# RWKV attention with two MoE layers on one core: r's odd columns read in place by the first level's matmuls, and the order of VectorE's steps changed

## What is computed

```python
for t in range(S):                       # attention with a decaying state
    cur = einsum('bhd,bhe->bhde', u * k[t], v[t])
    y[t] = einsum('bhd,bhde->bhe', r[t], state + cur)
    state = w[t][..., None] * state + einsum('bhd,bhe->bhde', k[t], v[t])
x = relu(y @ w_in) ** 2 @ w_out          # dense MLP, 384 -> 2048 -> 384
out = gate * (relu(x[e] @ w1[e]) @ w2[e])  # top-1 of 8 experts, 384 -> 1024 -> 384
```

## Time and profile before

| | |
|---|---|
| three runs, us | 453.21, 453.87, 456.42 (median 453.87) |
| the profiled execution, us | 453.21 |
| its span in the profile, us | 451.2 |
| mean granted clock of PE | 0.997 |
| DMA | 63.39 MB, mean 140 GB/s |

### The profile page before, as it was taken

The page is one execution under the profiler, slowest core; times in us unless marked ns, Lnnn a source line. Parts: engine busy times, 40 slices in busy tenths (PEclk is TensorE's granted clock), DMA queues, the critical chain, the costliest instruction groups (busy, mean ns, idle before and its releaser), DMA issues.

```text
span 451.2 us, 14525 instructions
## 1 busy us (share of the span) xinstructions
PE 427.7 (95%) x5882; PEld 405.8 (90%) x5882; DVE 303.3 (67%) x763; ACT 257.5 (57%) x527; POOL 57.1 (13%) x77
## 2 busy tenths in 40 slices
PE   2689999999999999999999999999999899999994
PEld 2578999999999999999999999998997789999994
DVE  4787956667777867786868638658548877677510
ACT  2265866446654665466556565574548876586421
POOL 7400000000000100010001000211030333321201
PEclk9999999999999999999999999999999999999998
DMA  8817795870220123000000085522885998520001
GB/s 275 290 52 257 275 315 204 286 303 4 98 99 3 37 74 124 1 26 15 3 3 20 21 293 199 175 89 67 308 266 156 333 336 277 195 62 2 30 2 44
DMA packets 35643, 63.39 MB, mean 140 GB/s; under 512 B 3981, under 2 KB 21951, under 8 KB 35569
## 3 DMA queue, kind: packets, MB, share of 16 engines
q1 hardware_dynamic: 33264, 57.88, 37.5%
q0 software_dynamic: 2304, 4.47, 2.7%
HBM read 50.77 MB, written 14.19 MB: 144 GB/s over the span
## 4 chain that ended last, share of the span: by engine, by line
PE 87%; issue 3%; DVE 3%; ACT 3%; DMA 3%; SPq 1%; POOLq 0%; DVEq 0%; ACTq 0%
PE bank L719 22%; PE bank L705 22%; PE pair L626 6%; PE bank L932 6%; PE bank L885 5%; PE pair L590 4%; PE pair L885 3%; PE pair L900 3%; PE bank L939 3%; PE bank L900 3%; PE pair L645 2%; PE pair L680 1%; DMA KS<-in_krw 1%; DMA stage<-in_moe_w_in 1%; PE pair L657 1%
## 5 line engine op out<-in xcount | busy, mean ns | idle before, releaser
L705 PE MATMUL bank<-XH,W 128*128 128x256 f32 x576 | 118.7, 284 | 0.1
L719 PE MATMUL bank<-W,GH 128*128 128x384 f32 x372 | 98.3, 345 | 0.0
L705 PEld LDWEIGHTS bank<-XH,W 128*128 128x128 f32 x576 | 94.9, 189 | 1.1 <-issue 0.4
L705 PE MATMUL bank<-XL,W 128*128 128x256 f32 x288 | 80.6, 280 | 0.0
L1277 DVE TENSOR_TENSOR GL<-GG,GH 128x256 fp32r<-128x256 f32 x96 | 40.3, 419 | 34.5 <-ACT GH L971 34.2
L1075 ACT ACTIVATE RB<-bank 128x256 f32<-128x256 f32 x96 | 36.6, 381 | 46.6 <-PE bank L705 46.0
L719 PEld LDWEIGHTS bank<-W,GH 128*128 128x128 f32 x372 | 61.7, 188 | 1.2
L719 PE MATMUL bank<-W,GL 128*128 128x384 f32 x186 | 62.6, 337 | 0.0
L971 ACT ACTIVATE GH<-GG 128x256 fp32r<-128x256 f32 x96 | 40.2, 418 | 34.8 <-PE bank L719 33.0
L1214 DVE TENSOR_TENSOR KS<-KS 128x512 f32<-128x512 f32 x72 | 49.6, 690 | 8.1 <-PE pair L626 8.0
L705 PEld LDWEIGHTS bank<-XL,W 128*128 128x128 f32 x288 | 54.3, 189 | 0.0
(11 more groups left out here) (164 smaller groups left out, 710.2 us busy)
## 6 DMA issues: line engine op xcount, KB each, us to landing
raw<-in_moe_w SPq DMA_DIRECT2D x23, 768.0 KB, 7.4
stage<-in_moe_w SPq DMA_DIRECT2D x9, 768.0 KB, 7.9
KS<-in_krw SPq DMA_DIRECT2D x12, 512.0 KB, 6.1
slots<-X SPq DMA_DIRECT2D x8, 579.0 KB, 6.3
VV<-in_v SPq DMA_DIRECT2D x12, 288.0 KB, 7.0
KS<-in_krw SPq DMA_DIRECT2D x12, 256.0 KB, 6.3
stage<-in_moe_w_in SPq DMA_DIRECT2D x4, 768.0 KB, 7.3
stage<-in_moe_w_out SPq DMA_DIRECT2D x4, 768.0 KB, 6.6
```

The costliest lines, as they stand in the source:

```text
L705: last = nc.tensor.matmul(bank[4 + f % 2][:, 0:2 * P], win[wa][:, c, f * P:(f + 1) * P], xa[:, c, :], start=n == 0, stop=n == 3 * KM - 1)
L719: last = nc.tensor.matmul(bank[6 + m][:, 0:DM], ga[(NF * g + f) % G3][:, cols], wout[wa][:, f, :], start=f == 0 and n == 0, stop=f == NF - ...
```

## The change

- `mixed_copied` copies only k's even columns into `MIX` (256 elements per partition). `first_level` takes as moving operand the 32 even columns of `UT` and then the 32 odd columns of r where they were loaded, so the first level's columns come out evens first, then odds; PE waits for the load as well.
- `first_select` writes `AD` and reads `eye` (now laid out [C / 2, 2]) with a stride of 2, to undo that order. POOL builds `eye` in two instructions.
- `update` of level 0 waits for the first level's matmuls (which still read r), so `first_select` stands ahead of it. `next_totals` goes into `update`, and `upd` is raised by the totals instead of by the update; DVE waits for `tot` only in block 0. The waits for `made` and `cleared` move ahead of the pipeline.
- `level` uses n = 64 stationary columns for levels 1 to 4 (32 for level 5, as before).

```diff
--- before.py
+++ after.py
@@ -115,7 +115,7 @@
         GL = [sb(f"GL{n}", [P, 2 * P], F32R, on=p1) for n in range(G3)]
         mask2 = IN[0][0][:, :, :].rearrange("p h n -> p (h n)")[:, 0:NMASK * C].rearrange("p (l n) -> p l n", l=NMASK)
         mask = sb("mask", [P, NMASK, C // 2], on=p1)
-        eye = sb("eye", [P, C], on=p1)
+        eye = sb("eye", [P, C // 2, 2], on=p1)
         U = sb("U", [P, HP], on=p1)
         empty = X2[:, 0, :]
         X2B = sb("X2B", [P, 2, ROW], on=p1)
@@ -355,10 +355,6 @@
             first = off[l] - off[1]
             return UT[t][i % 2][:, first:first + (XW >> l)] if l else KRW[t][i % 2][:, 2 * XW:3 * XW]
 
-        def every_second(first, apart):
-
-            return bass.AP(first.tensor, first.offset, [first.ap[0], [apart, 2], [2, XW // 2]])
-
         def left_right(x):
             return x.rearrange("p (g two o) -> p two g o", two=2, o=1)
 
@@ -507,11 +503,11 @@
                                                pattern=[[2 * L, C // L], [0, L]], channel_multiplier=-1)
             step(last)
             pool.wait_ge(cst, n_cst[0])
-            step(nc.gpsimd.tensor_tensor(eye[:, :], ident[:, 0:C], ident[:, C:P], ALU.add))
+            step(nc.gpsimd.tensor_tensor(eye[:, :, 0], ident[:, 0:C:2], ident[:, C:P:2], ALU.add))
+            step(nc.gpsimd.tensor_tensor(eye[:, :, 1], ident[:, 1:C:2], ident[:, C + 1:P:2], ALU.add))
             step(nc.gpsimd.tensor_tensor(mask[:, :, :], mask2[:, :, 0:C // 2], mask2[:, :, C // 2:C], ALU.add))
             pool.wait_ge(cst, n_cst[0])
-            odd = right_half(eye[:, :], 0)[:, :, 0]
-            nc.gpsimd.tensor_tensor(odd, odd, mask[:, 0, :], ALU.add).then_inc(made, 1)
+            nc.gpsimd.tensor_tensor(eye[:, :, 1], eye[:, :, 1], mask[:, 0, :], ALU.add).then_inc(made, 1)
 
             def first_totals(t, l):
 
@@ -600,6 +596,7 @@
 
             def first_level(i, t):
 
+                pe.wait_ge(ld_kr[t][i % 2], 16 * (i // 2 + 1))
                 pe.wait_ge(mixed_raw[t], i + 1)
                 pe.wait_ge(mixed_u[t], i + 1)
                 need(pe, xl_ready[t], i)
@@ -607,8 +604,10 @@
                     for h in range(2):
                         for a in range(2):
                             rows, c = slice(DP * a, DP * a + D), q * P + h * C
-                            last = nc.tensor.matmul(pair[t][half(h, a), a, q * P:q * P + C], MIX[t][rows, c:c + C],
-                                                    UT[t][i % 2][rows, c:c + C], start=q == 0, stop=q == HP - 1)
+                            even = UT[t][i % 2][rows, c:c + 1]
+                            reads = bass.AP(even.tensor, even.offset, [even.ap[0], [XW + 1, 2], [2, C // 2]])
+                            last = nc.tensor.matmul(pair[t][half(h, a), a, q * P:q * P + C], MIX[t][rows, c:c + C], reads,
+                                                    start=q == 0, stop=q == HP - 1)
                 last.then_inc(att[t], 1)
 
             def level(i, t, l):
@@ -617,7 +616,7 @@
                 if t == 0 and i >= 3 and l == NL - 1:
                     pe.wait_ge(rank_used, i - 2)
                 x = KRW[t][i % 2]
-                n = C - (1 << l)
+                n = C if l < NMASK else C // 2
                 for q in range(HP):
                     for h in range(2):
                         for a in range(2):
@@ -973,8 +972,7 @@
             def mixed_copied(i, t):
                 act.wait_ge(ld_kr[t][i % 2], 16 * (i // 2 + 1))
                 need(act, inc_done[t], i)
-                copy(every_second(UT[t][i % 2][:, 1:2], (2 - i % 2) * WIDTH - 1),
-                     every_second(KRW[t][i % 2][:, 1:2], XW - 1)).then_inc(mixed_raw[t], 1)
+                copy(MIX[t][:, 0:XW:2], KRW[t][i % 2][:, XW:2 * XW:2]).then_inc(mixed_raw[t], 1)
 
             def level_blocks(i, t):
                 act.wait_ge(att[t], NSTEP * i + NL)
@@ -1193,42 +1191,40 @@
 
                 dve.wait_ge(ld_kr[t][i % 2], 16 * (i // 2 + 1))
                 need(dve, inc_done[t], i)
-                out = every_second(UT[t][i % 2][:, 0:1], (2 - i % 2) * WIDTH + 1)
-                x = every_second(KRW[t][i % 2][:, 0:1], XW + 1)
-                tt(out.rearrange("p r (q n) -> p r q n", q=HP), x.rearrange("p r (q n) -> p r q n", q=HP),
+
+                def both(first, apart):
+                    return bass.AP(first.tensor, first.offset, [first.ap[0], [apart, 2], [P, HP], [2, C]])
+
+                tt(both(UT[t][i % 2][:, 0:1], (2 - i % 2) * WIDTH + 1), both(KRW[t][i % 2][:, 0:1], XW + 1),
                    U[:, :].rearrange("p (r q n) -> p r q n", r=1, n=1).to_broadcast([P, 2, HP, C]),
                    ALU.mult).then_inc(mixed_u[t], 1)
 
             def update(i, t, l):
                 L = 1 << l
+                n = XW // (2 * L)
+                dve.wait_ge(att[t], NSTEP * i + l + 1)
                 if l == 0:
                     dve.wait_ge(ld_wd[t][i % 2], 16 * (i // 2 + 1))
-                    dve.wait_ge(mixed_raw[t], i + 1)
                     dve.wait_ge(mixed_u[t], i + 1)
                 else:
-                    dve.wait_ge(att[t], NSTEP * i + l + 1)
                     dve.wait_ge(upd[t], NL * i + l)
-                    dve.wait_ge(tot[t], NL * i + l)
+                if i == 0:
+                    need(dve, tot[t], l)
+                td = left_right(totals(i, t, l))
                 x = halves(i, t, l)
-                td = left_right(totals(i, t, l))
-                tt(x, x, td.to_broadcast([P, 2, XW // (2 * L), L]), ALU.mult).then_inc(upd[t], 1)
-
-            def next_totals(i, t, l):
-
+                last = tt(x, x, td.to_broadcast([P, 2, n, L]), ALU.mult)
                 if i > 0:
-                    td = left_right(totals(i, t, l))
-                    tt(totals(i, t, l + 1), td[:, 0, :, 0], td[:, 1, :, 0], ALU.mult).then_inc(tot[t], 1)
+                    last = tt(totals(i, t, l + 1), td[:, 0, :, 0], td[:, 1, :, 0], ALU.mult)
+                last.then_inc(upd[t], 1)
 
             def first_select(i, t):
 
                 dve.wait_ge(att[t], NSTEP * i + 1)
-                if i == 0:
-                    dve.wait_ge(made, 2)
-                    dve.wait_ge(cleared, 2)
+                got = pair[t][:, :, :].rearrange("p a (q c) -> p (a q) c", q=HP)[:, :, 0:C]
                 nc.vector.copy_predicated(
-                    AD[t][:, :, :],
-                    eye[:, :].bitcast(U32).rearrange("p (x n) -> p x n", x=1).to_broadcast([P, H, C]),
-                    pair[t][:, :, :].rearrange("p a (q c) -> p (a q) c", q=HP)[:, :, 0:C]).then_inc(sel[t], 1)
+                    AD[t][:, :, :].rearrange("p x (n b) -> p x b n", b=2),
+                    eye[:, :, :].bitcast(U32).rearrange("p (x n) b -> p x b n", x=1).to_broadcast([P, H, 2, C // 2]),
+                    got.rearrange("p x (b n) -> p x b n", b=2)).then_inc(sel[t], 1)
 
             def select(i, t, l):
                 L = 1 << l
@@ -1251,14 +1247,17 @@
             def scale_start(i, t):
 
                 if not opens(i, t):
-                    dve.wait_ge(tot[t], NL * (i + 1))
+                    dve.wait_ge(upd[t], NL * i + NL)
+                    if i == 0:
+                        dve.wait_ge(tot[t], NL)
                     need(dve, end_ready, 2 * i + t)
                     tt(heads(SD[:, :]), heads(start_state(i, t)), decay(i, t, 0), ALU.mult).then_inc(mid_scaled, 1)
 
             def state(i, t):
                 n = 2 * i + t
                 dve.wait_ge(inc_ready[t], i + 1)
-                dve.wait_ge(tot[t], NL * (i + 1))
+                if i == 0:
+                    dve.wait_ge(tot[t], NL)
                 if not opens(i, t):
                     dve.wait_ge(mid_scaled, n + 1 - opened(i, t))
                     tt(states(i, t)[:, 0], SD[:, :], states(i, t)[:, 0], ALU.add).then_inc(mid_ready, 1)
@@ -1402,13 +1401,10 @@
                 if (n, t, k) == (0, 0, 0):
                     mixed_weighted(0, 1)
                 if k == 0:
-                    update(n, t, k)
                     first_select(n, t)
-                else:
-                    if k < NMASK:
-                        select(n, t, k)
-                    update(n, t, k)
-                next_totals(n, t, k)
+                elif k < NMASK:
+                    select(n, t, k)
+                update(n, t, k)
 
             def body(i, attn, mlp, gate):
                 for s in range(NF):
@@ -1463,6 +1459,8 @@
                 nc.vector.memset(AD[t][:, :, :], 0.0).then_inc(cleared, 1)
             dve.wait_ge(ld_u, 16)
             mixed_weighted(0, 0)
+            dve.wait_ge(made, 2)
+            dve.wait_ge(cleared, 2)
             pipeline(dve, body)
 
             def first_rows_low(q):
```

## The result

The changed kernel takes 458.49 us in the median of 14 runs, the kernel before 453.99 beside it: the ratio is 1.0091, with a 95% interval of 1.007 to 1.0111, so some 4.1 us more (the two medians are 4.5 apart). The profiled execution took 458.81 us with a span of 457.1 and a mean granted clock of PE of 0.996, against 0.997 before, so the clock is not what differs.

The account below looks back on a forecast made before the run. PE was taken as the bound, holding 87% of the chain. Terms of 1.7 (columns), 0.14 (block 1's later signal) and 0 gave +1.84: 455.1 us against the profile's 453.2, 455.7 on the median; range 452.8 to 458.7.

Parts of the forecast that it names:

- the forecast case: Whole kernel: 1.84 us more, 455.7 us on the median, 0.4% longer; chance 0.55.
- Rival A: First select on DVE: strided select costs double, PE waits 0.5 us in blocks 2 to 5; 458.2 us, chance 0.13.
- edit 1: Levels 1 to 4 on PE: 64 stationary columns take 1.06 us a level, 0.35 a block, 1.7 us in all.
- The estimate of 8 us in all: Levels 1 to 4 weight loads, by the skill's columns divided by 1.2 ns: 1.6 us a block, 8 in all.
- rivals B: Levels 1 to 4 on PE: 64 columns run at the increments' pace, 0.93 us; 453.1 us, chance 0.15.
- D: Levels 1 to 4 on PE: loads serialise, each level about twice its 0.85 us; 468 us, chance 0.03.
- edit 2: First level and ACT's copies: r's odd columns read where loaded, copy halved; worth 0, upper bound 0.8 us.
- edit 3: DVE's order: select, update, totals, later upd; 0 in steady state and block 0, +0.14 us in block 1.
- the margin of 0.7 us: Level 1 of t=1, steady state: DVE's totals done at 83.0, PE arriving at 83.74, so no wait.
- The 0.14 in block 1: Block 1, chain from DVE's update to PE: upd raised by the totals comes 0.14 us later.
- edit 4: First select on DVE with stride 2 in AD and eye: stays at 0.73 us, upper bound 1.33.
- Rival C: PE's instruction stream: an uncaused stall of 1.8 us vanishes (453.9) or a second appears (457.5); chance 0.14, both directions.

Follow-up runs that it names:

- b1: Changed kernel with the earlier 62, 60, 56 and 48 stationary columns in levels 1 to 4; ratio 1.0065 to the kernel before.
- e4: Kernel before with one edit, 64 stationary columns in levels 1 to 4; ratio 1.0027 to the kernel before.
- e2: Changed kernel, first select walking AD and eye contiguously with the stride on its PSUM operand; ratio 1.0036 to the kernel before.
- c1: Changed kernel with the select's stride on PSUM and the earlier short stationary columns; ratio 1.0002 to the kernel before.
- e1: Changed kernel, first level's moving operand taking even and odd columns in turn, so the select needs no stride; ratio 1.0052 to the kernel before.
- e3: Changed kernel with eye laid out in reading order, so only AD is strided; select 1319 ns, one execution, no ratio.
- b2: Changed kernel with upd raised by the update itself and DVE waiting for tot again; ratio 1.0064 to the kernel before.
- d1: Kernel before with the first select walking all three operands evens first (stride 2), old DVE order; ratio 1.0018 to the kernel before.

## Why the prediction was right or wrong

The time lies in the range, 0.2 us from its upper end, and within 1% of before, as forecast. But the forecast case, 1.84 us more, didn't come; 4.1 were measured. Rival A came, with a chance of 0.13, almost to the number: 458.2 predicted for it, 458.5 measured. That the time lies in the range is owed to A's place in it, and A's total is in part luck, as its share in block 0 shows below.

- **The columns (edit 1)** were right: 1.06 a level was taken, 1.06 is measured in level after level; 1.7 us was the term (level 3's row of 0.99 was one with a record missing; its others are 0.96, so 0.38 a block), 1.2 (b1), 1.2 (e4) and 0.0034 x 454 = 1.5 (e2 against c1) are what the runs give. The estimate of 8 us in all from the figure of the Trainium skill ("TensorE: Matmul & The Clock Gate", section on LDWEIGHTS) is refuted by the 1.06; so are rivals B (0.93) and D.
- **Reading r in place (edit 2)** is worth 0, and so is ACT's smaller copy, by c1 and within its interval. The stride of 8 bytes in the moving operand costs nothing (the first level takes 1.10 in c1). e1 shows that this isn't so for every access pattern.
- **DVE's order (edit 3)** was right as far as the sum went: with a select of 0.73, PE waits for DVE nowhere in blocks 2 to 5 (e2, c1), and the margin of 0.7 us is 0.6 in e2 (totals done at 84.19, PE's second half at 84.83). The 0.14 in block 1 came as worked out. Rival A's sum had PE wait 0.5 us a block; in block 2 it was 0.43, and 186.73 - 185.10 = 1.6 over four blocks says 0.4.
- **The strided select (edit 4)** is the step that failed, a term that was mis-sized: taken as nothing, with a select of 0.73 us, it measured 1.31 and 2.5 to 2.9 us of the whole. I took 0.73 because `mixed_weighted` walks with stride 2 for nothing, and read the dear select of level 1 as an effect of an innermost loop of two. e2 has such a loop and takes 738 ns; the changed kernel and e3 have a loop of 32 and take 1313 and 1319. What they have in common with level 1's select is that the *predicated* copy writes fewer than four neighbours at a time. The upper bound, 0.73 + 2 x 0.30 = 1.33, was worked out from exactly that row and was the value. A row of the same operation should have counted for more than a row of another operation with the same stride.
- **Block 0**: PE's second wait for instructions ended 0.54 later where A had 0.5, but counted from DVE's start it was 1.1. Ahead of the steady state the slow select seems to cost more than A's 0.5: the products of block 1 begin at 65.17 to 66.42 us in the five kernels with the fast select (before, e1, e2, e4, c1) and at 66.60 to 67.24 in the five with the slow one (changed, e3, b1, b2, d1), 1.2 us apart in the mean. The weight DMA of the earlier trace rows lands at 41.75 to 43.00 in the first five and at 43.19 to 43.87 in the others. How the select would delay it no run isolates, and each is one execution. A's sum was 0.5 + 2.0 for the select and 1.84 for the rest; the runs give about 1.2 + 1.6 and 1.5, so its parts missed in opposite directions.
- **Rival C**: PE's stalls without a cause stand where they were; the one ahead of an expert (L899) is 1.7 us instead of 1.8. No wait of over 1 us came or went between the two profiles.
- What I had not seen: GL, which now comes later, makes ACT's squaring wait (5.3 us in eight places in blocks 2 to 5). PE's waits in those blocks name only the totals (1.2 us in four places), so nothing is seen to follow from it. The waits of the blocks and the time ahead of them make 4 x 0.4 + 1.2 = 2.8 us, beside the 2.5 that separate the changed kernel from e2 and the 2.9 between b1 and c1; the differences are within the intervals.

Together: 2.5 us for the select, 1.5 for the columns, 0.1 for all the rest (c1). These are steps from the changed kernel over e2 and c1 to before, so they make up the 4.1 by construction; what confirms them is b1 - c1 (2.9) for the select and b1 and e4 (1.2 each) for the columns.

## What to carry to other kernels

When a reordering leaves one operand with a stride, try the stride on each of the others: here it was free on PSUM and nearly doubled the instruction on the written side. A new order can cost nothing (c1), a slow instruction little (d1), and the two together 2.9 us (b1); the margin has to be worked out with both. Work that is taken off an engine that nobody waits for (ACT's copies here) pays for nothing, so it can't stand against even 1.5 us on the engine that bounds.

## What the runs showed of the hardware

- A predicated copy on DVE of 128 x 512 elements takes 732 to 745 ns when it writes contiguously and 1310 to 1319 when it writes every second element; a stride on its PSUM operand (32 elements, two at a time) changes nothing (738), nor does taking the stride off its mask (1319 against 1313). The Trainium skill ("SBUF — State Buffer", in "Door 1: The DMA port swizzle", the note on cachelines) lets 4 fp32 be strided over for free, and an ordinary multiply that writes with stride 2 agrees (0.69 us for 512); the predicated copy doesn't. Why it alone is slower no run here shows.
- Level 1's select, which writes runs of two, goes with the strided one; runs of four and more don't. From 256 to 512 elements the time grows from 0.43 to 0.73 us with runs of four or more, 1.2 ns an element, and from 0.74 to 1.31 with runs of two and of one, 2.2 ns.
- A first level whose moving operand jumps between two places at each element takes 1.50 us, against 1.09 with two strided runs of 32.
- Stationary columns cost little but not nothing in the levels: 48, 56, 60, 62 and 64 columns take 0.85, 0.96, 1.01, 1.04 and 1.06 us for 64 pairs of load and MATMUL. With 64 columns every one of levels 1 to 4 takes 1.06 where nothing delays it (changed kernel, e4), so it is the columns and not the level.
- ACT's copy of 256 elements with stride 2 takes 438 ns where one of 512 took 672, so some 200 ns are not proportional to the elements.
